# Attention scores from plain fp32 matmuls over 64 rows, in place of a high and a low part

## What is computed

```python
scores = scale * np.matmul(q, k.transpose(0, 1, 3, 2))        # scale = 1/sqrt(64)
thresh = np.max(scores, axis=-1, keepdims=True) - tau
scores = np.where(scores >= thresh, scores, -1000000000.0)
scores = scores - np.max(scores, axis=-1, keepdims=True)
attn = np.exp(scores)
attn = attn / (np.sum(attn, axis=-1, keepdims=True) + 1e-09)
x = np.matmul(attn, v)                                        # to (batch, seq, 512)
u = x + mixing over the positions of rank 32                  # second stage
x = u + relu(u @ w_ch1) @ w_ch2
out = (sigmoid(conv(x)) * (x @ w_val)) @ w_out                # third stage
```

## Time and profile before

| | before |
|---|---|
| median of 3 runs | 890.07 us (887.07 to 891.19) |
| span of the profiled execution (first to last instruction of the program) | 888.5 us |
| PE busy (matmul) | 857.3 us, 96% |
| PEld busy (weight loads) | 787.6 us, 89% |
| DVE, ACT, POOL busy | 447.1, 386.6, 408.5 us |
| scores, L283 and L284, first to last start | 8.3 to 312.1 us |

### The profile page before, as it was taken

How to read it: one execution, slowest core, us unless ns; L and a number is a source line. 1 busy time by engine, 2 the same in 40 slices (tenths; PEclk the granted TensorE clock), 3 DMA queues, 4 the chain that set the end, 5 groups by cost and what they waited for, 6 DMA issues and landing times. The chain is left out here.

```text
span 888.5 us, 19413 instructions
## 1 busy us (share of the span) xinstructions
PE 857.3 (96%) x7104; PEld 787.6 (89%) x7104; DVE 447.1 (50%) x981; ACT 386.6 (44%) x933; POOL 408.5 (46%) x306
## 2 busy tenths in 40 slices
PE   5999999999999989999999999999999999859998
PEld 4888888888888859999999999999999999859897
DVE  6888888888888855311241122411233131592331
ACT  5888888888888833221111211112112121432431
POOL 5997777667771020056083550835509164470000
PEclk9999999999999999999999999999999999979999
DMA  7544333433332002300000000000000100212311
GB/s 171 120 107 107 78 78 101 112 100 78 78 78 76 12 13 84 84 1 27 1 1 27 2 28 2 1 27 1 27 1 1 51 24 28 101 52 76 113 63 72
DMA packets 27734, 49.03 MB, mean 55 GB/s; under 512 B 5344, under 2 KB 14112, under 8 KB 27680
## 3 DMA queue, kind: packets, MB, share of 16 engines
q1 hardware_dynamic: 24944, 43.54, 18.2%
q10 hardware_dynamic: 2736, 4.72, 1.4%
HBM read 38.81 MB, written 8.85 MB: 54 GB/s over the span
## 5 line engine op out<-in xcount | busy, mean ns | idle before, releaser
L847 DVE SCALAR_TENSOR_TENSOR h_lo<-psum,h_hi 128x288 fp32r<-128x288 f32 x128 | 58.6, 458 | 297.4 <-ACT h_hi L787 297.4
L787 ACT ACTIVATE h_hi<-psum 128x288 fp32r<-128x288 f32 x128 | 52.7, 412 | 262.5 <-PE psum L725 262.5
L723 PE MATMUL psum<-u_split,w_hi 128*128 128x288 f32 x512 | 158.6, 310 | 4.2 <-PEq L165 3.1
L724 PE MATMUL psum<-u_split,w_hi 128*128 128x288 f32 x512 | 152.9, 299 | 0.0
L725 PE MATMUL psum<-u_split,w_lo 128*128 128x288 f32 x512 | 152.9, 299 | 0.0
L738 PE MATMUL psum<-h_lo,w_hi 128*128 128x288 f32 x512 | 151.0, 295 | 0.0
L739 PE MATMUL psum<-h_hi,w_lo 128*128 128x288 f32 x512 | 150.9, 295 | 0.0
L737 PE MATMUL psum<-h_hi,w_hi 128*128 128x288 f32 x512 | 150.6, 294 | 0.0
L498 DVE TENSOR_REDUCE neg_max<-psum 128x1 f32<-128x576 f32 (+1 forms) x160 | 120.7, 754 | 28.7 <-PE psum L284 25.1
L507 DVE SCALAR_TENSOR_TENSOR probs<-psum,thresh,exp_scores 128x576 f32<-128x576 f32 (+1 forms) x160 | 128.1, 801 | 0.8 <-ACT exp_scores L398 0.8
L283 PE MATMUL psum<-qk_split 128*128 128x288 f32 (+1 forms) x320 | 106.7, 348 | 10.4 <-DVE qk_split L486 9.4
(11 more groups left out here) (108 smaller groups left out, 1568.1 us busy)
## 6 DMA issues: line engine op xcount, KB each, us to landing
qk_raw<-in_qk SPq DMA_DIRECT2D x60, 288.0 KB, 4.8
out<-o_sb ACTq DMA_DIRECT2D x18, 256.0 KB, 2.0
w_stage<-in_w SPq DMA_DIRECT2D x16, 256.0 KB, 2.7
v_main<-in_v SPq DMA_DIRECT2D x16, 256.0 KB, 2.7
conv<-in_w SPq DMA_DIRECT2D x16, 256.0 KB, 2.6
conv_dram<-conv SPq DMA_DIRECT2D x7, 576.0 KB, 2.8
gates<-conv_dram SPq DMA_DIRECT2D x7, 576.0 KB, 3.8
probs<-in_qk SPq DMA_DIRECT2D x4, 288.0 KB, 4.8
```

The source lines that it names most:

```text
L723: nc.tensor.matmul(out, w1_hi[:, cols], u_hi[:, half, d], start=(d == 0), stop=False)
L724: nc.tensor.matmul(out, w1_hi[:, cols], u_lo[:, half, d], start=False, stop=False)
```

## The change

The scores are made by two plain fp32 matmuls in a block in place of four fp32r ones. The first takes q and k from the partitions 0 to 63 and makes the first 288 keys, the second takes them from 64 to 127 and makes the other 288. Nothing is split any more: the tiles `split` and `k_lo` are gone, and POOL scales q alone. `raw` now has room for three pairs (six heads), loads go up to three pairs ahead and wait for PE's scores (`s_ready`) in place of POOL's splitting, with one semaphore for each of the three places. The first pair is loaded into `raw` too, and DVE scales its q once all four of its loads have landed. `evacuate_tokens` has one wait less. (Lines cut are marked.)

```diff
-    raw = sb("qk_raw", [P, 2, 2, S])
-    split = sb("qk_split", [P, 6, 2, S], F32R)
-    k_lo = sb("k_lo", [P, 6, S], F32R)
+    raw = sb("qk_raw", [P, 6, 2, S])
...
             def load(p, t):
                 pair = index(p, t)
-                for a in range(2):
-
-                    wait(sp, split_ready, 2 * p + a - 3, 2 * BODY_PAIRS, t)
-                    if p > 1:
-                        for h in range(2):
-                            sp.dma_start(raw[D * h:D * h + D, a], qk[pair * 2 + a]).then_inc(qk_in[a], 16)
+                if p > 1:
+                    load_heads(p, t)
...
+            def load_heads(p, t):
+
+                wait(sp, s_ready, 2 * QB * (p - 2), 2 * BODY, t)
+                for a in range(2):
+                    for h in range(2):
+                        sp.dma_start(raw[D * h:D * h + D, (2 * p + a) % 6], qk[index(p, t) * 2 + a]
+                                     ).then_inc(qk_in[p % 3], 16)
...
-            for a in range(2):
-                for h in range(2):
-                    sp.dma_start(probs[D * h:D * h + D, a].rearrange("p (a b) -> p a b", a=2),
-                                 qk[a]).then_inc(first_in[a], 16)
-            for a in range(2):
-                for h in range(2):
-                    sp.dma_start(raw[D * h:D * h + D, a], qk[2 + a]).then_inc(qk_in[a], 16)
+            for p in range(2):
+                load_heads(p, None)
...
             def work(p, t):
+                wait(pool, qk_in[p % 3], 64 * (p // 3 + 1), 64, t)
                 for a in range(2):
...
-                    nc.gpsimd.tensor_tensor(hi, raw[:, a], one[:].unsqueeze(2).broadcast_to([P, 2, S]),
-                                            ALU.mult).then_inc(part_done, 1)
...
-                    nc.gpsimd.tensor_tensor(k_lo[:, hd % 6], k_in, hi[:, 1].bitcast(F32),
-                                            ALU.subtract).then_inc(part_done, 1)
...
-                    nc.gpsimd.tensor_tensor(hi[D:P, 0], q_in[D:P], hi[D:P, 0].bitcast(F32),
-                                            ALU.subtract).then_inc(split_ready, 1)
+                    q_in = raw[:, (2 * p + a) % 6, 0]
+                    nc.gpsimd.tensor_tensor(q_in, q_in, q_scale[:].broadcast_to([P, S]), ALU.mult).then_inc(q_scaled, 1)
                 if p > 1:
-                    wait(pool, split_ready, 2 * p, 2 * BODY_PAIRS, t)
                     w1_low(p - 2, t)
...
                     cols = slice(h * HALF, (h + 1) * HALF)
-                    nc.tensor.matmul(out, split[:, hd, 0, rows], split[:, hd, 1, cols], start=True, stop=False)
-                    mm = nc.tensor.matmul(out, split[:, hd, 0, rows], k_lo[:, hd, cols], start=False, stop=True)
+                    part = raw[D * h:D * h + D, hd]
+                    mm = nc.tensor.matmul(out, part[:, 0, rows], part[:, 1, cols], start=True, stop=True)
                 mm.then_inc(s_ready, 1)
...
-            for hd in range(2):
-                act.wait_ge(first_in[hd], 32)
-                nc.scalar.copy(split[:, hd, 1], probs[:, hd, S:2 * S]).then_inc(first_hi, 1)
-                act.wait_ge(q_scaled, hd + 1)
-                nc.scalar.copy(split[:, hd, 0], probs[:, hd, 0:S]).then_inc(first_hi, 1)
...
+            dve.wait_ge(qk_in[0], 64)
             for hd in range(2):
...
+                nc.vector.tensor_scalar(raw[:, hd, 0], raw[:, hd, 0], q_scale[:], None, ALU.mult).then_inc(first_scaled, 1)
...
-                    dve.wait_ge(split_ready, B * H - 2)
```

More of the change, by code:

```diff
@@ L133, in attention @@
     tau_in = sem("tau_in"); one_ready = sem("one_ready")
-    qk_in = [sem(f"qk_in{i}") for i in range(2)]
+    qk_in = [sem(f"qk_in{i}") for i in range(3)]
     v_in = [sem(f"v_in{i}") for i in range(3)]
-    first_in = [sem(f"first_in{i}") for i in range(2)]
     w1_in = sem("w1_in")
@@ L139, in attention @@
     zero_ready = sem("zero_ready")
-    q_scaled = sem("q_scaled"); first_hi = sem("first_hi"); first_split = sem("first_split"); part_done = sem("part_done"); split_ready = sem("split_ready")
+    first_scaled = sem("first_scaled"); q_scaled = sem("q_scaled")
     s_ready = sem("s_ready"); max_done = sem("max_done"); exp_done = sem("exp_done")
@@ L226, in work @@
             def work(p, t):
+                wait(pool, qk_in[p % 3], 64 * (p // 3 + 1), 64, t)
                 for a in range(2):
[L228 to L242, removed]
-                    nc.gpsimd.tensor_tensor(hi, raw[:, a], one[:].unsqueeze(2).broadcast_to([P, 2, S]),
-                                            ALU.mult).then_inc(part_done, 1)
-                    wait(pool, part_done, parts + 2, 6 * BODY_PAIRS, t)
-                    nc.gpsimd.tensor_tensor(k_lo[:, hd % 6], k_in, hi[:, 1].bitcast(F32),
-                                            ALU.subtract).then_inc(part_done, 1)
-                    wait(pool, part_done, parts + 3, 6 * BODY_PAIRS, t)
-                    nc.gpsimd.tensor_tensor(hi[D:P, 0], q_in[D:P], hi[D:P, 0].bitcast(F32),
-                                            ALU.subtract).then_inc(split_ready, 1)
+                    q_in = raw[:, (2 * p + a) % 6, 0]
+                    nc.gpsimd.tensor_tensor(q_in, q_in, q_scale[:].broadcast_to([P, S]), ALU.mult).then_inc(q_scaled, 1)
                 if p > 1:
-                    wait(pool, split_ready, 2 * p, 2 * BODY_PAIRS, t)
                     w1_low(p - 2, t)
@@ L273, in score_rows @@
                 if b == 0 and t is None and pair == 0:
-                    pe.wait_ge(first_split, a + 1)
+                    pe.wait_ge(first_scaled, a + 1)
                 elif b == 0:
-                    wait(pe, split_ready, 2 * pair + a - 1, 2 * BODY_PAIRS, t)
+                    wait(pe, q_scaled, 2 * pair + a - 1, 2 * BODY_PAIRS, t)
                 wait(pe, probs_done, n - 2, 2 * BODY, t)
@@ L547, in evacuate_tokens @@
             def evacuate_tokens(k):
-                if k == 0:
-                    dve.wait_ge(split_ready, B * H - 2)
                 dve.wait_ge(tok_ready, k + 1)
```

## The result

The changed kernel takes 905.19 us (median of 4 runs, 904.39 to 906.52); the kernel before takes 890.46 us in 4 runs. The ratio is 1.0177 with a 95% interval of 1.016 to 1.0194: slower by 14.7 us. The profiled execution has a span of 903.4 us against 888.5, so 14.9 us more, and was timed at 905.14, 1.7 us above its span. A few runs hundreds of us longer than the others of the same kernel (one of e10_before_spread_dve, two of the kernel before taken beside e4, e5, e6 and e8) are left out of all figures here.

What follows compares the result with a forecast made beforehand. The prediction took PE's own chain of 160 score blocks to bound the attention: 888.5 us of span + 16.6 for longer blocks - 0.9 at the start = 904.2, with the median 1.6 above, 905.8 us; range 893 to 945.

Steps and rivals of the forecast that it cites:

- What bounds the kernel: Attention's steady part: PE's own chain of 160 score blocks bounds it, every ns counts; POOL's savings count only at the start.
- the sum: Score block of 128 rows after the change: 0.11 load + 0.484 + 0.09 + 0.06 = 0.744 us, +0.104; times 160, +16.6 us.
- Plain fp32 cost: Score matmuls: 0.84 ns a column and record, so 0.242 us for a record of 288 columns, four a block.
- The row halves run side by side: Score block: the two 64-row matmuls overlap fully, like L322's column halves, so four records take 0.484 us.
- B: Score block: program order, second half starts with the first half's second record; 38.7 us more, 944.5 us; chance 0.10.
- C: Score block: row halves don't overlap at all, two records more a block; 983.2 us; chance 0.08.
- The change of form: Behind each score block, leaving the 64-row form: 0.09 us pause plus 0.06 uncovered load, 0.15 together.
- D: Behind the score block: leaving the 64-row form costs nothing, block 0.046 us less than now; 881.8 us; chance 0.07.
- E: Behind the score block: of the 0.15 only the load's 0.06 us stays, nearly no change; 891.4 us; chance 0.07.
- The start: First blocks: first maximum at about 10.3 us, 0.9 earlier; between 0 and -1.2 us in all, -0.9 taken.
- The waits moved: Steady part: PE's wait at L276 becomes one for POOL's scaling of q, met early; PE stays without waits.
- The total: Whole kernel: 888.5 + 16.6 - 0.9 = 904.2 us of span, median 1.6 above it, 905.8 us.

Runs made afterwards that it cites:

- e10_before_spread_dve: Kernel before, reciprocals of both heads transposed in one full-form matmul, DVE spreading them by a copy behind the second weights: 875.0 us (0.9827).
- e4: Changed kernel, DVE taking reciprocals spread over 64 columns a head, PE transposing both heads in one full-form matmul: 898.1 us (1.009).
- e5: Kernel before, DVE taking reciprocals spread over 64 columns a head, PE transposing both heads in one full-form matmul: 887.8 us (0.9977).
- e6: Changed kernel, the first head's two loads given their own semaphore, so DVE scales its q without waiting for all four: 905.3 us (one run).
- e8: Changed kernel, a step's two score blocks together and DVE's widened reciprocals transposed in one full-form matmul: 990.0 us (1.112).
- e3_pool_back: Changed kernel, POOL again doing the three splitting operations of every head from pair 1 on, into tiles nobody reads: 904.9 us (1.0167).
- e1: Changed kernel, both matmuls of a score block reading the copy in partitions 0 to 63, so one row half: 990.8 us (1.113).
- e2: Changed kernel, both matmuls of a block taking all 128 rows in full form, with q's scale halved: 957.0 us (1.075).
- e7: Changed kernel, PE taking a step's two score blocks one right behind the other, ahead of the transposes: 936.0 us (1.0518).
- e9: Kernel before, reciprocals of both heads transposed in one full-form matmul, DVE taking two columns and ACT spreading them: 869.25 us (0.9771).

## Why the prediction was right

**What bounds the kernel:** right. PE was full before and is full after; +0.107 us a block in the steady part against 0.104 in the sum, because every ns of PE's chain counts. POOL's 149 us were worth nothing (e3_pool_back).

**Plain fp32 cost:** right. 0.242 us for a record of 288 columns; e1 and e2 show four in a row in 1.14 and 1.07 us with what lies around them.

**The row halves run side by side:** right. It was carried over from L322's column halves, and e1 shows its worth, 0.478 us a block, both records of one half. Rivals B and C would have left less or nothing to lose there. The Trainium skill's rule on program order (TensorE: Matmul & The Clock Gate, Part 3), by which 944.5 came out, does not give the time of this kernel: two records of each block start together from its first one on, though in the code one matmul stands behind the other. Whether the rule itself fails stays open, as no view tells in what order the built program holds the four records.

**The change of form:** right in size, 0.15 predicted, 0.146 by e2 against e1. Its parts were 0.09 and 0.05 to 0.06 in the timeline. D rested on all of this being free, E on the 0.09.

**The start:** right in sum (0.8 us earlier, 0.9 predicted), less so in its steps. The first maximum came at 10.66, not 10.3, as the last of four loads released DVE at 8.62 where 8.44 was assumed. And the chain of waits from the first maximum on is not the whole reason. PE's records come down to their later distances at about 19 us in the profile before and at about 17 us in the one after. In e3_pool_back, with the same start as the changed kernel, it was 19 us, and the first mark stood 0.3 us later (18.6). So part of the 0.8 is luck, of the one execution that was profiled.

**The waits moved:** right. PE's wait for the scaled q never shows, and POOL waits for loads, not PE for POOL.

The total, 905.8 against 905.19, has an error of 0.6 us that is smaller than its parts deserve: the steady part came out near the sum (16.5 us over 154 blocks, 16.6 predicted for all 160), and the start and the scatter of the later stages, 0.8 each, happened to be no more than this. What the sum did not have in it, and e7, e5 and e8 show, is how near DVE stands: the forecast was easy to make because the change only lengthened PE's chain. The same arithmetic applied to shorten it missed by 24 to 111 us in these three, where DVE's place in a ring of waits, or its own price, had been taken as slack. It missed by 4 in e4 and landed in e9, where DVE kept its short reciprocal.

## What to carry to other kernels

Cost a matmul by the distance of neighbouring starts, and look in the trace for whether two tiles start together before counting on array tiling: here plain fp32 in two 64-row halves costs 0.73 us a block, 1.07 in the full form, 0.64 with the operands split for fp32r. Count the changes of array form in a step (each 0.09 us of pause and 0.05 to 0.11 of uncovered load): an edit that took two of them out gave more (21 us) than the change of this document took (15). When PE gets shorter, re-read the second engine: 14% of idle time on DVE was not room for another 0.8 us in each step, nor for a tighter order.

## What the runs showed that was not expected

The reciprocal on DVE: 0.154 us for 2 columns, 0.94 us for 128, while a copy of 128 columns takes 0.25 us there and 0.30 on ACT.

The records of PE at the start are twice as far apart as later: 0.48 us for a plain fp32 record of 288 columns in e1, where the block at 20.21 takes 2.21 us to its transposes. The windows of most runs read a granted clock of 1.00 there, and that reading is not to be trusted: in three runs (e3, e7, e8) they read 0.50 in a part of this stretch, and the distances go with it. In e7_blocks_together they fall to the later ones at 13.4 us, double again at 16.3, and fall for good at about 23. Two of its blocks and two windows (0.50 is 1.2 GHz):

```profile
14.80 0.76 PE L259 MATMUL psum<-qk_raw 64*128 64x288 f32 x4 [0.65 <-DVE probs L470]
16.26 1.33 PE L259 MATMUL psum<-qk_raw 64*128 64x288 f32 x4 [0.71 <-DVE probs L470]
13.00:15.00 2.00, 0.96 (x6) 0.50 (x8) 2.00 (x6) 1.33 (x4) 1.18 (x2) 1.00 1.13 298
16.00:22.00 6.00, 4.97 (x21) 2.99 (x23) 3.27 (x9) 3.08 (x9) 0.28 (x2) 0.50 1.03 217
```

The four records of a block cover 0.76 us at 1.00 and 1.33 at 0.50. Until when the distances are double differs from profile to profile: about 19 us before, 17 in the changed kernel, 19 in e3, 20 in e6, 23 in e7, 30 in e1. So the first blocks are best priced from rows of the start, with some us of play, and the clock is best read there from the distances.
